# Expert stage of an attention, MoE, MoE kernel: down products two tiles behind the up products, row numbers ahead of pads, low-row scaling split, last tiles apart

## What is computed

```python
noisy_logits = x @ w_gate + np.log1p(np.exp(x @ w_noise)) * noise
top2 = np.argpartition(-noisy_logits, 2, axis=1)[:, :2]
...
for e in range(E):
    for k in range(2):
        mask = top2[:, k] == e
        h = np.maximum(x[mask] @ w1[e], 0.0)
        out[mask] += top2_w[mask, k, None] * (h @ w2[e])
```

## Time and profile before

| | |
|---|---|
| three executions | 992.29, 998.05, 998.0 us; median 998.0 us |
| the profiled execution | 997.57 us by the clock of the runs, its span 995.9 us |
| granted TensorE clock, mean over the span | 0.987 of full speed |
| PE busy | 958.7 us, 96% of the span |
| DVE, ACT, POOL busy | 522.2, 328.5, 501.9 us |
| the chain that ended last | PE 81%, DMA 7%, DVE 5%, POOL 2% |
| DMA | 145.99 MB, mean 147 GB/s |

### The profile page before, as it was taken

The page is one execution under the profiler, slowest core; times in us unless marked ns, Lnnn a source line. Parts: engine busy times, 40 slices in busy tenths (PEclk is TensorE's granted clock), DMA queues, the critical chain, the costliest instruction groups (busy, mean ns, idle before and its releaser), DMA issues.

```text
span 995.9 us, 18444 instructions
## 1 busy us (share of the span) xinstructions
PE 958.7 (96%) x5864; PEld 847.1 (85%) x5865; DVE 522.2 (52%) x942; ACT 328.5 (33%) x453; POOL 501.9 (50%) x715
## 2 busy tenths in 40 slices
PE   6999999999999999999989999999989999999995
PEld 6999999999999999999767687788867888888883
DVE  5564555555556556664746544455444545544354
ACT  3533333333333332332313333333323333333231
POOL 5991001001001001598578868588784879803354
PEclk9999999999999999999899999999999999999998
DMA  8622323423433423744667657667676675448639
GB/s 338 244 75 74 89 92 108 111 100 106 107 107 107 90 92 122 235 152 135 203 159 179 176 130 169 169 137 179 152 163 149 169 162 122 95 95 174 174 101 322
DMA packets 193895, 145.99 MB, mean 147 GB/s; under 512 B 159920, under 2 KB 160048, under 8 KB 193840
## 3 DMA queue, kind: packets, MB, share of 16 engines
q1 hardware_dynamic: 175360, 89.94, 36.0%
q0 software_dynamic: 12288, 44.05, 14.0%
q10 hardware_dynamic: 6192, 11.27, 3.0%
HBM read 65.80 MB, written 40.63 MB: 107 GB/s over the span
## 4 chain that ended last, share of the span: by engine, by line
PE 81%; DMA 7%; DVE 5%; POOL 2%; issue 2%; SPq 1%; ACT 1%; POOLq 0%; DVEq 0%; ACTq 0%
PE ps L1343 21%; PE ps L1445 18%; PE ps L1330 18%; PE ps L1357 14%; PE ps L1361 7%; DMA hT_halves<-h_halves 5%; POOL y_hi L599 2%; PE ps L1371 1%; PE ps L1299 1%; PE ps L1278 1%; DVE hT_part L1227 1%; ACT hT_part L772 1%; DVE h_halves L1213 1%; DVE hT L1221 1%; DMA y_hi<-routed_y,y_rows 1%
## 5 line engine op out<-in xcount | busy, mean ns | idle before, releaser
L1445 PE MATMUL ps<-W,hT_part 128*128 (+1 forms) x1032 | 252.6, 401 | 13.8 <-DVE hT_part L1227 12.0
L1330 PE MATMUL ps<-W,xg_part 128*128 (+1 forms) x1032 | 252.2, 399 | 3.8 <-DVE xg_part L990 3.8
L1445 PEld LDWEIGHTS ps<-W,hT_part 128*128 128x128 f32 x1032 | 197.1, 192 | 63.3 <-issue 17.5
L1330 PEld LDWEIGHTS ps<-W,xg_part 128*128 128x128 f32 x1032 | 195.1, 190 | 51.1 <-issue 4.1
L1343 PE MATMUL ps<-x_part,W 128*128 128x384 f32 x1152 | 221.7, 341 | 0.5 <-DVE x_part L862 0.5
L1343 PEld LDWEIGHTS ps<-x_part,W 128*128 128x128 f32 x1152 | 200.9, 188 | 2.7 <-POOL W L511 0.7
L558 POOL TENSOR_TENSOR W<-EXraw,W 128x256 fp32r<-128x256 f32 x224 | 189.8, 878 | 4.7
L521 POOL DMA_INDIRECT routed_x<-x_halves,slot_blk x30 | 29.6, 988 | 300.8 <-DVE slot_blk L945 292.2
L1357 PE MATMUL ps<-g_part,W 128*128 128x384 f32 x768 | 150.6, 338 | 0.0
L1357 PEld LDWEIGHTS ps<-g_part,W 128*128 128x128 f32 x768 | 134.8, 188 | 0.3 <-ACT g_part L649 0.2
L554 POOL TENSOR_SCALAR W<-EXraw 128x256 fp32r<-128x256 f32 x224 | 107.6, 505 | 42.1 <-PE ps L1330 35.1
(11 more groups left out here) (181 smaller groups left out, 743.2 us busy)
## 6 DMA issues: line engine op xcount, KB each, us to landing
EXraw<-in_w POOLq DMA_DIRECT2D x24, 1024.0 KB, 6.6
QKV<-qkv SPq DMA_DIRECT2D x15, 768.0 KB, 4.4
routed_y<-y_sb ACTq DMA_DIRECT2D x43, 256.0 KB
routed_y<-zero_tile SPq DMA_DIRECT2D x14, 768.0 KB, 4.0
Wraw<-w_moe SPq DMA_DIRECT2D x16, 512.0 KB, 10.3
EXraw<-in_w SPq DMA_DIRECT2D x8, 1024.0 KB, 5.6
out<-y_lo SPq DMA_DIRECT2D x18, 256.0 KB
routed_x<-zero_tile SPq DMA_DIRECT2D x8, 256.0 KB, 2.1
```

The lines of the kernel that those rows point to most:

```text
L1330: last = nc.tensor.matmul(dst, a(ha), b(hb), start=(opens and i == 0), stop=(closes and i == n - 1))
L1445: last = nc.tensor.matmul(ps[:, 4, :], hT_part[hh][:, n, :], W[hw][:, weights(slot, W1W + n * DM, DM)], start=(n == 0 and k == 0), stop=(n ...
```

## The change

PE's loop becomes `expert_up(g)`, `expert_down(g-2)`: each down product has one more product ahead of it. ACT and DVE get the matching order: `turned_high(g-1)`, `turned_low(g-1)` and `take_y(g-2)` now stand ahead of `merge(g)` in step g. All steps from 3 to 41 are turned by DMA; only the last (42) is turned by PE, into tiles of its own (`h_last`, `hT_last`), and the down products 40, 41 and 42 have their own PSUM banks (4, 5, 6). `h_residual` and its matrix are gone. In `tile_tables` the steps for `row_tab` come first, with a semaphore of their own (`row_ready`); SP loads three row numbers at once and issues the turns of tiles 3 and 4 ahead of the five last pads. At the end a third of the `y_lo` tiles is scaled by ACT, and DVE's last `take_y` stands between its scaling and its adding.

```diff
@@ SP
             for p in range(3):
                 pad(p)
-            sp.wait_ge(tab_ready, 1)
+            sp.wait_ge(row_ready, 1)
+            rows = [row_of(g) for g in range(EARLY, 2 * EARLY)]
             for n in range(2):
                 sp.wait_ge(scattered_late[n], SCATTERS)
             sp.wait_ge(spare_stored, 16)
             for g in range(EARLY, 2 * EARLY):
                 for p in range((0, 2, 3)[g - EARLY], (2, 3, E)[g - EARLY]):
                     sp.wait_ge(padded[p], 16)
-                turn_x(g)
-                if g == EARLY:
+                turn_x(g, rows[g - EARLY])
+                if g == EARLY + 1:
                     for p in range(3, E):
                         pad(p)
@@ ACT
             def turned_tile(g, first=False):
                 halve(g, first)
                 xg_high(g + 1)
+                if not first:
+                    turned_high(g - 1)
+                    store_y(g - 2)
                 merge(g)
-                turned_high(g)
-                store_y(g - 1)
...
+            act.wait_ge(wmix_ready, 2)
+            for r in range(ABREAST):
+                act.wait_ge(lo_got[r], 16 * T // ABREAST)
+            for t in range(2, T, 3):
+                nc.scalar.mul(y_lo[t][:], y_lo[t][:], wmix[:, t, 0:1]).then_inc(lo_scaled_scalar, 1)
+            store_y(GL)
@@ DVE
+            def turned_tile(g, first=False, more=True):
+                if first:
+                    xg_low(g + 1)
+                    halve(g, first)
+                else:
+                    halve(g)
+                    xg_low(g + 1)
+                if more:
+                    merge_x(g + 2)
+                if not first:
+                    take_y(g - 2)
+                    turned_low(g - 1)
                 merge(g)
-                take_y(g - 1)
-                turned_low(g)
...
             for t in range(T):
-                nc.vector.tensor_scalar(y_lo[t][:], y_lo[t][:], wmix[:, t, 0:1], None, ALU.mult).then_inc(lo_scaled, 1)
+                if t % 3 < 2:
+                    nc.vector.tensor_scalar(y_lo[t][:], y_lo[t][:], wmix[:, t, 0:1], None, ALU.mult).then_inc(lo_scaled, 1)
+            take_y(GL)
@@ PE
             expert_up(EARLY, tell=True)
-            expert_down(EARLY - 1)
             with pe.Fori(EARLY + 1, GL - 1) as g:
                 expert_up(g, turned=True, tell=True)
-                expert_down(g - 1)
-            pe.wait_ge(minus_ready, 1)
-            for g in range(GL - 1, G):
-                expert_up(g, between=(lambda g=g: h_residual(g - 1)) if g > GL else None, turned=g == GL - 1)
-                expert_down(g - 1)
-                hidden_transpose(g)
-            h_residual(G - 1)
-            expert_down(G - 1)
+                expert_down(g - 2)
+            expert_up(GL - 1, turned=True, tell=True)
+            expert_down(GL - 3)
+            expert_up(GL, turned=True)
+            expert_down(GL - 2, between=lambda: hidden_transpose(GL))
+            expert_down(GL - 1)
+            expert_down(GL)
```

More of the change, by code:

```diff
@@ L482, in _ @@
                 turn_x(g + EARLY)
-            turn_x(G - 1)
+            for g in range(G - EARLY, GL):
+                for s in range(2):
+                    turn_half(g, s)
             for t in range(T):
@@ L776, in turned_tile, with end_high @@
                 xg_high(g + 1)
+                if not first:
+                    turned_high(g - 1)
+                    store_y(g - 2)
                 merge(g)
-                turned_high(g)
-                store_y(g - 1)
             turned_tile(EARLY, first=True)
-            with act.Fori(EARLY + 1, GL - 1) as g:
+            with act.Fori(EARLY + 1, GL) as g:
                 turned_tile(g)
-            def hidden_rest(g):
-                act.wait_ge(h_rest, g - GL + 1)
-                nc.scalar.copy(hT_part[LO][:], ps[:, 2:4, :].rearrange("p a (n c) -> p (a n) c", c=P)).then_inc(hl_ready, 1)
-            def copy_y(g):
-                act.wait_ge(y_ready, g + 1)
-                act.wait_ge(y_stored, 16 * g)
-                nc.scalar.copy(y_sb[:], ps[:, 4, :]).then_inc(y_taken, 1)
-            for g in range(GL - 1, G):
-                if g > GL:
-                    hidden_rest(g - 1)
-                hidden(g)
-                if g + 1 < G:
-                    xg_high(g + 1)
-                if g > GL:
-                    copy_y(g - 1)
-                store_y(g - 1)
-                hidden_high(g)
-            hidden_rest(G - 1)
-            copy_y(G - 1)
-            store_y(G - 1)
+            def end_high(g, a):
+                for s in range(2):
+                    act.wait_ge(merged[s], g - EARLY + 1)
+                if a == 0:
+                    act.wait_ge(down_half, 1)
+                else:
+                    act.wait_ge(y_ready, g)
+                part = slice(a * KF // 2, (a + 1) * KF // 2)
+                nc.scalar.activation(hT_part[HI][:, part, :], hT[:, part, :], ACT.Relu).then_inc(end_hi, 1)
+            hidden(GL)
+            end_high(GL - 1, 0)
+            hidden_high(GL)
+            end_high(GL - 1, 1)
+            store_y(GL - 2)
+            store_y(GL - 1)
+            act.wait_ge(wmix_ready, 2)
[4 more added lines that the diff above has]
+            store_y(GL)
             act.wait_ge(y_stored, 16 * G)
@@ L1399, in up_half, with expert_up @@
                 return product(ps[:, s, :], terms, range_of_k[0] == 0, range_of_k[-1] == KD - 1)
-            def h_residual(g):
-                pe.wait_ge(hh_ready, g + 1)
-                for a in range(2):
-                    last = nc.tensor.matmul(ps[:, 2 + a, :], minus[:], hT_part[HI][:, 4 * a:4 * a + 4, :].rearrange("p n c -> p (n c)"),
-                                            start=False, stop=True, skip_group_check=True)
-                last.then_inc(h_rest, 1)
-            def expert_up(g, between=None, turned=False, tell=False):
+            def expert_up(g, turned=False, tell=False):
                 slot = expert_slot(g)
@@ L1415, in expert_up @@
                 for s in range(F2 // BANK):
-                    if s > 0 and between is not None:
-                        between()
                     if turned:
@@ L1436, in expert_down @@
                     pe.wait_ge(ex_down_ready, need)
-                pe.wait_ge(hh_ready, g + 1)
-                pe.wait_ge(hl_ready, g + 1)
-                if not isinstance(g, int) or g > 0:
+                static = isinstance(g, int)
+                rows = hT_last if static and g == GL else hT_part
+                if static and g == GL:
+                    pe.wait_ge(last_hi, 1)
+                    pe.wait_ge(last_lo, 1)
+                elif not static or g < GL - 1:
+                    pe.wait_ge(hh_ready, g + 1)
+                    pe.wait_ge(hl_ready, g + 1)
+                if not static or 0 < g <= GL - 2:
                     pe.wait_ge(y_taken, g)
                 for n in range(KF):
-                    if between is not None and n == KF // 2:
+                    if between is not None and n == at_n:
                         between()
+                    if static and g == GL - 1 and n % (KF // 2) == 0:
+                        pe.wait_ge(end_hi, n // (KF // 2) + 1)
+                        pe.wait_ge(end_lo, n // (KF // 2) + 1)
                     for k, (hh, hw) in enumerate(PASSES):
-                        last = nc.tensor.matmul(ps[:, 4, :], hT_part[hh][:, n, :], W[hw][:, weights(slot, W1W + n * DM, DM)],
+                        last = nc.tensor.matmul(ps[:, y_bank(g), :], rows[hh][:, n, :], W[hw][:, weights(slot, W1W + n * DM, DM)],
                                                 start=(n == 0 and k == 0), stop=(n == KF - 1 and k == 2))
+                    if static and g == GL - 2 and n == KF // 2 - 1:
+                        last.then_inc(down_half, 1)
                 last.then_inc(y_ready, 1)
```

106 lines of the change are left out of this document (63 added, 43 removed).

## The result

The changed kernel took 982.45 us (median of 981.44 to 984.22, four executions), against 996.56 us (992.29 to 998.05, four) of the kernel before: ratio 0.9867, 95% interval 0.9831 to 0.9903. That is not all of it. Two later sets, on two chips, with 22 executions of the changed kernel and 58 of the one before, gave 1.0053 (1.0030 to 1.0076) and 1.0019 (0.9986 to 1.0052): slower by half a per cent in one, no difference in the other. The ratios leave out executions more than 1.5% above the fastest of the same kernel; medians and ranges count them. The profiled execution of the first set took 984.22 us, its span is 982.7 us.

What follows compares the result with a forecast made beforehand. PE, busy 96% of the span, was taken as the bound. Down product 39 ending at 939.3 us plus a tail of 46 gave 985.3 of span, plus 1.7 outside it: 987.0 us against 997.57, range 979 to 995.

Steps and rivals of the forecast that it cites:

- The loop: PE's steps from down product 4 to the end of down product 39: 414.06 us becomes 402.5, 11.6 us gained.
- The start: Ahead of the loop: up product 3 0.85 us earlier, the point comparable with 537.64 at 536.8, gain 0.8 us.
- The open term: Whether 1.6 us of idle PE before up product 4 brings the lower clock; taken as no, costing 1.6 us otherwise.
- The end: Copy, stores, gathers and additions after down product 39: 46 us instead of 44.2, 1.8 us longer.
- POOL's descriptors don't get out while DVE is dense: In the tail, DVE's dense scalings and additions hold gathers; the 18th goes out at D + 37 instead of D + 34.0.
- D: The moment down product 39 ends, forecast at 939.3 us instead of 951.70.
- Its signs: In the tail's profile: two or more gathers of y_hi as long as DVE's runs, the last addition near 981.5.
- The first rival: Tail: additions do not hold POOL; 18th gather at D + 28.6, last store D + 40.3, 981.3 us; chance 0.25.
- the last result copy waits for down 42 at D + 23.3: In the tail, DVE's last result copy waits for down product 42 until D + 23.3; additions start at D + 24.
- the four cases: Whole kernel: 987 us (chance 0.40), 981 us (0.25), 992 us (0.31), or slower, 1012 us (0.04).
- half eaten by new waits: Slow clock before up products 4 and 5, one or two loop waits: 3 to 7 us lost, 992 us; chance 0.31.

Runs made afterwards that it cites:

- the start edits: Kernel before with only the earlier row-number tables and loads, tile 4 turned ahead of five pads, ranks one piece earlier: 992.32 us against 988.35, ratio 1.0046.

## Why the prediction was right, and where it was not

987.0 us forecast, 982.45 measured in the set that it was made for, inside 979 to 995, and faster by 1.3% where 1.1% was said. Part of this agreement is luck: the four executions of the kernel before in that set took 992 to 998 us, while its medians in the larger sets are 987.39 to 992.22, and the late signal, which took the gain away in two other sets, did not come.

- **The loop** was right in kind and size: 402.5 us forecast from 537 to the end of down product 39, 402.56 measured, no bracket of idle left. Its premise about the kernel before was too firm. The sum took 16.3 us of waits and slow clock from one profile as the price of the old order. The run without loads shows that they go with meetings of turnings and weight loads, and the profiles of the old order price them from about 1 us (1.2 us of waits behind 537.6 with the start edits) to 16. So the gain is real where they fall badly, and nearly nothing where they don't.
- **The start**: up product 3 at 504.32 (504.8 forecast), up 4 at 513.59 (513.7). The open term fell on the bad side: behind its wait of 1.93 us came the lower clock, 1.65 us. Up product 5 did not wait, where 0.7 us was said. Down product 39 ended at 940.15, 0.85 us later than forecast.
- **The end** held the step that failed: "POOL's descriptors don't get out while DVE is dense". It put the 18th gather at D + 37; it went out at D + 25.7, and the tail took 42.6 us instead of 46. The step took for certain what happens to some gathers: in the old order one was held to the end of the additions in three of the four profiles with 18 scalings, in the changed kernel none. Its signs, two or more gathers as long as DVE's runs and a last addition near 981.5, did not come (the longest took 1.28 us, the last addition was over at 975.98). The first rival, in which DVE's additions bound the end, had the mechanism of this execution (last one over at D + 35.8, 36.4 forecast), but 4 us for the last store where 6.7 were needed: SP's queue was busy with the eighteen stores of 256 KB until 978.63, 2.6 us behind the last addition, and a store took about 4 us to land. By the Trainium skill, "SBUF — State Buffer", section "Who interferes with whom", DVE in a two-port mode, which a `tensor_scalar` can enter, blocks GpSimd for the whole instruction, while one with two SBUF inputs contends only with GpSimd's reads. The 0.33 us by which two gathers grew under the twelve scalings, of 0.40 us each, are no more than one such instruction. On the additions the traces don't agree with the page: most gathers pass them with 1.02 us, but three were held to their end (4.37, 6.36 and 6.36 us).
- **Not seen at all**: that the additions stand behind waits for products of spare rows, and what such a wait can cost. The step "the last result copy waits for down 42 at D + 23.3" named the place and took the arrival of a signal for granted. On two chips it came 8.5 to 8.7 us late in the unchanged version, and there the change gained nothing. None of the four cases held this. The times there, 991.38 and 992.03 us, are those of "half eaten by new waits" (992), but for another reason: that case sought its waits at the start and in the loop, and down product 39 ended at 939.54 and 940.83.

## What to carry to other kernels

Before a wait is priced from one profile, take a second one: if it stands at other tiles, it is a meeting of transfers, its price is a spread, and giving the transfer more time (a step more of distance) removes the spread rather than a fixed sum. Check what the engine that ends last has queued ahead of its last work; work nobody needs, here the copies of spare tiles, should not stand ahead of work that is needed, and its own stores can still be the last to land. And when a change moves which side waits in the tail (rows for additions, or additions for rows), look for the next bound at once: here it was the gathers and stores.

## What was not expected of the hardware

A transposing DMA of 128 x 1024 two-byte numbers takes 3.3 to 3.8 us from the end of its input to its use in half of the steps or more; with 1 MB loads issued near it, it took up to 9.8 us, and without these loads at most 5.2 us in the loop. An indirect gather beside a dense run of DVE took 1.0 to 1.5 us to issue in most cases, but seven of them ended only with the run, the longest after 6.36 us. With the indirect gathers running, a semaphore of PE came 8.5 to 8.7 us after its matmul, and in other versions 11.4 to 13.4 us after, in the sets on two chips; in one execution without the gathers it didn't. And an idle PE of 2.13 us ahead of up product 3 left the next group at 5.87 us (granted clock 1.00), while 1.76 us ahead of up product 4, in the same execution, was followed by 7.40 us (0.77):

```profile
504.58 5.87 PE L1372 MATMUL ps<-W,xg_part 128*128 x24 [2.13 <-DVE xg_part L1013]
512.21 7.40 PE L1372 MATMUL ps<-W,xg_part 128*128 x24 [1.76 <-DVE xg_part L1013]
```

so the length of the idle time alone does not say whether the clock falls.
